# A fused linear attention, routed experts and a feed-forward layer: scatters moved behind GpSimd's mask in three rounds, one sum of logits moved behind the queries

## What is computed

```
state = alpha[t] * state + k[t] (outer) v[t];   y[t] = q[t] @ state      # attention, per head
logits = normalised(x) @ normalised(emb).T / tau;   e = argmax(logits)
x = gate_weight * (relu(x @ w1[e]) @ w2[e])                              # one expert per token
h = x @ w_in;   out = where(h > 0, h, exp(min(h, 0)) - 1) @ w_out
```

## Time and profile before

| quantity | value |
|---|---|
| median of 3 runs | 894.9 us |
| the profiled execution: its time, and its span | 891.97 us, 890.3 us |
| PE busy | 867.2 us, 97% of the span |
| DVE, ACT, POOL busy | 49%, 37%, 32% of the span |
| granted TensorE clock | 0.998 of full speed |
| attention | from the start to about 166 us |
| first two expert tiles | about 166 to 190 us |

### The profile page before, as it was taken

One profiled execution on the slowest core, in us unless ns is written; L12 is line 12 of the kernel. 1 busy time (PEld: TensorE's weight loads), 2 busy tenths in 40 slices (PEclk: granted clock), 3 DMA queues, 4 the chain that ended last, 5 costly groups with the idle time before them and its releaser, 6 DMA issues. The chain is left out here.

```text
span 890.3 us, 16092 instructions
## 1 busy us (share of the span) xinstructions
PE 867.2 (97%) x5725; PEld 774.7 (87%) x5725; DVE 433.6 (49%) x810; ACT 326.7 (37%) x698; POOL 284.2 (32%) x276
## 2 busy tenths in 40 slices
PE   8999999899999999999999999999999999999996
PEld 6888887689989998998988989899989999899985
DVE  7889898752232232232226445445445445445442
ACT  4576667732223222222222323233223323233322
POOL 3235655464755574285517102002002002002001
PEclk9999999999999999999999999999999999999999
DMA  9976774778778878757517002002002002000001
GB/s 151 164 145 127 175 155 104 271 237 283 232 245 274 297 206 270 244 153 212 161 54 234 16 1 72 0 1 72 1 1 72 1 1 72 1 0 31 7 1 36
DMA packets 140575, 106.35 MB, mean 119 GB/s; under 512 B 103338, under 2 KB 129058, under 8 KB 140498
## 3 DMA queue, kind: packets, MB, share of 16 engines
q0 software_dynamic: 24896, 62.95, 22.3%
q1 hardware_dynamic: 115602, 42.37, 21.3%
HBM read 87.94 MB, written 17.35 MB: 118 GB/s over the span
## 5 line engine op out<-in xcount | busy, mean ns | idle before, releaser
L1463 POOL DMA_INDIRECT out<-of,idi x24 | 26.8, 1115 | 364.0 <-ACT of L1569 300.8
L1276 PE MATMUL bank<-WX,hdTh 128*128 (+1 forms) x496 | 128.7, 340 | 0.5 <-PEq L448 0.5
L1505 PE MATMUL bank<-xT_h,wi_h 128*128 128x512 f32 x288 | 114.1, 396 | 0.0
L1505 PE MATMUL bank<-xT_l,wi_h 128*128 128x512 f32 x288 | 113.6, 395 | 0.0
L1505 PE MATMUL bank<-xT_h,wi_l 128*128 128x512 f32 x288 | 113.3, 393 | 0.0
L1575 ACT ACTIVATE ee<-bank 128x512 f32<-128x512 f32 x96 | 57.5, 599 | 146.7 <-PE bank L1505 144.6
L1597 DVE TENSOR_SCALAR em<-ee 128x512 f32<-128x512 f32 x96 | 44.2, 460 | 136.3 <-ACT ee L1575 134.8
L1260 PE MATMUL bank<-WX,xdTh 128*128 (+1 forms) x372 | 99.7, 403 | 3.6 <-ACT xdTh L1304 2.0
L1578 ACT ACTIVATE g_h<-gg 128x512 fp32r<-128x512 f32 x96 | 60.7, 632 | 114.9 <-DVE gg L1602 113.2
L1195 POOL TENSOR_TENSOR WX<-raw_w,WX 128x3072 fp32r<-128x3072 f32 x14 | 95.6, 6830 | 15.9 <-DMA WX<-moe_w 12.6
L1606 DVE TENSOR_TENSOR g_l<-gg,g_h 128x512 fp32r<-128x512 f32 x96 | 68.5, 713 | 60.3 <-ACT g_h L1578 59.4
(11 more groups left out here) (215 smaller groups left out, 1442.0 us busy)
## 6 DMA issues: line engine op xcount, KB each, us to landing
WX<-moe_w POOLq DMA_DIRECT2D x13, 1536.0 KB, 9.8
raw_w<-moe_w POOLq DMA_DIRECT2D x13, 1536.0 KB, 7.7
xd<-sorted_x SPq DMA_DIRECT2D x31, 193.0 KB, 5.3
sorted_y<-yd SPq DMA_DIRECT2D x31, 192.5 KB, 4.1
xg<-sorted_y SPq DMA_DIRECT2D x6, 770.0 KB, 4.6
nat_a<-alpha SPq DMA_DIRECT2D x32, 144.0 KB, 4.2
nat_k<-k SPq DMA_DIRECT2D x32, 144.0 KB, 3.5
nat_q<-q SPq DMA_DIRECT2D x32, 144.0 KB, 4.5
```

The costliest lines, as they stand in the source:

```text
L1276: last = pe.matmul(y_out(t)[:, 0:DM], hdT[a][:, k * P:(k + 1) * P], WX[:, bass.ds(off + (b * WE + KD * F + k * DM), DM)], start=(k == 0 an ...
L1505: last = pe.matmul(bank[4 + i % 2][:, :], a[:, k, w], b[:, k, :], start=(k == 0 and m == 0), stop=(k == KD - 1 and m == 2))
```

## The change

In rounds 8 and 12, three scatters stood between `Gm` and the mask `M1`. Now one stands there, and the other two behind `Zm`, which is behind `M1`. In round 14, two scatters stood ahead of `M1`; now one does, and five are behind `Gm` instead of four. In round 14 DVE adds the logits of pair 13 behind `Qh1` of pair 15 instead of between `Kh1` and the states. PE, ACT and SP keep their order.

```
             if n == PAIRS - 2:
-                out_ = [("M0", n)] + [(x, n + 1) for x in ("G", "Kh0", "Kh1")] + [("LA", n - 1)] + sums
-                out_ += [(x, n + 1) for x in ("R", "F", "Qh0", "Qh1")] + [("Y8", PARTIAL - 1)]
+                out_ = [("M0", n)] + [(x, n + 1) for x in ("G", "Kh0", "Kh1")] + sums
+                out_ += [(x, n + 1) for x in ("R", "F", "Qh0", "Qh1")] + [("LA", n - 1), ("Y8", PARTIAL - 1)]
...
                 elif b == PARTIAL - 1 and r == 2:
...
-                    out_[0:0] = [("SC", b * C + j) for j in range(2)]
-                    out_ += [("SC", b * C + j) for j in range(2, C)] + [(f"X{i}", b) for i in range(X_STEPS)]
+                    out_[0:0] = [("SC", b * C)]
+                    out_ += [("SC", b * C + j) for j in range(1, C)] + [(f"X{i}", b) for i in range(X_STEPS)]
...
                 elif b < PARTIAL - 1 and r == 4:
                     i = place_of(out_, "M1")
-                    out_[i:i] = [("SC", b * C + j) for j in range(HC, C)]
+                    out_[i:i] = [("SC", b * C + HC)]
+                    i = place_of(out_, "Zm") + 1
+                    out_[i:i] = [("SC", b * C + j) for j in range(HC + 1, C)]
```

## The result

The changed kernel takes 899.87 us (median of five runs, 898.46 to 900.37); the kernel before took 895.15 us beside it (five runs, 894.73 to 895.42). The ratio is 1.0046, with a 95% interval from 1.0036 to 1.0057. The prediction was 893.1 us, between 892.0 and 895.1, with a chance of 0.04 for slower. It was wrong in sign: the measured change is a loss of 4.7 us by the medians and of 4.1 by the ratio.

What follows compares the result with a forecast made beforehand. TensorE, busy 97% of the span, was taken as the bound, with gains only from its waits or later starts. Terms of 0.61, 0.53 and 0.67 us took the median from 894.9 to 893.1 us, range 892.0 to 895.1.

Steps and rivals of the forecast that it cites:

- I count the wait of round 14 and `LA` at nothing for the end: Round 14: removing PE's wait for the mask and moving the logits' sum were counted as no gain at the end.
- attention may end earlier without moving it: The expert phase hangs on batch 2's last scatter (160.16 us), so attention ending earlier does not shift it.
- Rounds 8 and 12 (-0.61, -0.53): From `KV` to the next `KT`, PE gets back its mask waits: 0.61 us in round 8, 0.53 in round 12.
- Round 14, mask and `LA`: Mask, held by `G`, ends at 153.54 instead of 154.55; `F` starts at 155.40 instead of 156.06.
- The last scatter of batch 2 (-0.67): Round 14: third scatter passes ahead of `F`, fourth is held, the last starts at 159.49, 0.67 us earlier.
- caught by `F`: Rival: `F` holds round 14's third scatter, the last starts 0.59 us later; 894.35 us, chance 0.26.
- that of the second scatter: Rival: states and `F` keep out round 14's second scatter, the last starts 1.85 us later; 895.6 us, chance 0.08.
- the wait of about 3 us that I took as room for the gain: ACT idles 3.06 us for a weight DMA ahead of `Wc`; 0.67 of it goes, so the shift has room.

Runs made afterwards that it cites:

- before again: The kernel before, unchanged, profiled a second time: 895.49 us (11 runs), ratio 1.0002, span 893.9.
- `LA` alone: Only the sum of the logits of pair 13 moved behind the queries, against the kernel before: 895.31 us (11 runs), ratio 0.9999.
- the run that was to part the two: The changed kernel with 24 more matmuls on TensorE between `KT0` and `A0` of pair 15: 898.6 us (7 runs), ratio 1.004.

## Why the prediction was wrong

**The step that failed.** "I count the wait of round 14 and `LA` at nothing for the end", together with "attention may end earlier without moving it". The prediction followed moved scatters only into GpSimd's queue, `Gm` and the token loads, and gave the hand-offs from TensorE to the other engines no cost. The runs show 3.89 us from `KT` of pair 15 to `A` instead of 1.39, and 3.59 us more from `A` to the first expert tile, and all of it with round 14's scatters.

**Rounds 8 and 12 (-0.61, -0.53).** The steps were right up to the mask: it starts inside `F`, is held (1.66 and 1.65 us; I expected about 1.9), and no `Yi1` waits. The size was mis-read from one execution. In the second profile of before, `KV` to `KT` takes 3.65 us in both rounds already (97.31 to 100.96, 137.22 to 140.87), with no wait for the mask: there is nothing to give back at that place. The time is lost earlier, at ACT's copy `C1`. Round 8 in the second profile of before, and in the changed kernel:

```profile
93.62 0.81 ACT L956 ACTIVATE asb<-bank 128x768 f32<-128x768 f32 x1 [2.07 <-PE bank L713]
```

```profile
92.85 0.81 ACT L958 ACTIVATE asb<-bank 128x768 f32<-128x768 f32 x1 [1.34 <-PE bank L658]
```

In the second profile of before, two scatters of round 8 run freely between `Gm` and `F` (91.50 and 92.79, `F` at 93.02), and `C1` starts 1.07 us behind the end of `A`. In the changed kernel one does, and it is 0.33. This is lateness again. It holds in both rounds of every profile: `C1` waits 2.04 to 2.15 us in the three with two free scatters there (before again, round 14's scatters alone, `LA` alone), and 1.05 to 1.61 in the ten in which the change leaves one. The first profile of before had one free scatter too, because `F` held the second (92.73, 2.20 us), and waited 1.33.

The change moves the two scatters to where ACT waits for the states. In the changed kernel `KV` to `KT` takes 5.11 us in round 8 (95.62 to 100.73) and 4.37 in round 12 (135.66 to 140.03), not 3.6: ACT's states start 1.57 and 0.80 us behind the end of `KV`, with the moved scatters running (95.87 and 97.18, 135.90 and 137.21), and `Ys` waits for them or for DVE. Round 11, where nothing was moved, takes 4.37 in the changed kernel and 4.21 in the second profile of before, against 3.60 in the earlier trace rows. In all, against that second profile, scan `G` of round 14 starts 0.84 us earlier in the changed kernel (153.72 against 154.56), where 1.14 was forecast.

**Round 14, mask and `LA`.** Right in size: the mask ends 0.67 us after `G` (154.44 + 1.69 against 155.46; predicted 0.66), and `F` starts 4.27 us behind `G` (153.72 to 157.99) instead of 4.93 in the second profile of before: 0.66 earlier, as predicted. Most of it comes from the mask: with the scatters of round 14 alone and `LA` still ahead of the states, it is 4.35 (154.55 to 158.90). What fell is that this counts for nothing at the end. I asked what `Yi1` and `F` gain, not what moving a scatter between the scans does to everybody else.

**The last scatter of batch 2 (-0.67).** Right in mechanism: the third scatter passes, 0.22 us ahead of `F` (157.77 and 157.99, predicted 0.23), the fourth is held (159.03 + 1.48 = 160.51, 0.76 us behind `F`'s end; predicted 0.77), and the last starts 8.37 us behind `G` instead of 9.02 (162.09; 163.58 in the second profile of before), 0.65 us earlier. So the rival "caught by `F`" did not happen, nor that of the second scatter, which took 0.99. With the 0.84 us of the rounds ahead the last scatter is 1.49 us earlier, and the token loads follow: 165.01 instead of 166.56, 1.55 us earlier where 1.81 was forecast. But "attention may end earlier without moving it" had an unspoken other half: attention may not end *later*. It did. `Wc` starts at 177.16 without any wait for the DMA; the wait of about 3 us that I took as room for the gain was consumed by attention.

**What made it slower** was none of the rivals. In the second profile of before, `F` held one scatter for its whole length:

```profile
159.60 2.41 POOL L1050 DMA_INDIRECT sorted_x<-xb,slot  x1 [0.30 <-issue]
```

So there one scatter (158.31) runs freely between the mask and `F`. In the changed kernel two do, because the third now starts just ahead of `F`, which is exactly what the term of -0.67 counted as its gain. PE's steps `Ys`, `Tq`, `KT` of round 14 are then seen late, while `F` is over. The loss by rows: from `KT` of pair 15 to `A` 3.89 us instead of 1.39, +2.50. From `A` to the first expert tile 14.08 instead of 10.49, +3.59; of this 2.5 us are `A` (2.93 against 1.61), `KV` (1.31 against 0.79) and `YN` (1.65 against 0.94) at the low clock. Less the 1.49 us by which `KT` came earlier (159.08 against 160.57), the first expert tile is 4.60 later. The span is 3.5 longer: PE's wait of 1.1 us for ACT in that tile, which the second profile of before has, is gone.

**What is shown and what isn't.** Shown: the loss is all in round 14's scatters (1.0042 alone, 0.9997 without them). With at most one scatter running freely between the mask and `F` the stall ahead of `A` doesn't arise (both profiles of before, the change without round 14, the scatters of rounds 8 and 12 alone, `LA` alone, the two variants that hold or delay the third, and the two that move all five away); with two it does (five kernels); and with the third held, the lateness follows the scatters to their new place (two kernels). TensorE's earlier arrival is not the cause: in all of these `KT` starts 1.08 to 1.14 us behind `F`, stall or not. By single runs: taking the weight load away doesn't remove the stall, and plain transfers of the same rows don't bring it. Only argued: how much of the loss would go if the clock stayed up, since the run that was to part the two missed. Open: why scatters that follow each other delay what others see of TensorE, and why the first profile of before was spared in rounds 7 and 11, with the same scatters at the same times (two free ones, 86.29 and 87.84, against 86.35 and 87.89). So the number of free scatters alone doesn't decide it everywhere. Whether TensorE's signal itself is late or its last writes are can't be told from rows that say "remote". Not tried: scatters further apart in rounds 7 to 12, where the lateness stands in before as well.

## What to carry to other kernels

An operation that is blocked may be doing the others a service: before filling the gap ahead of a long vector operation with one more indirect DMA, ask which cross-engine hand-offs of TensorE fall into that stretch, and whether they have the slack to come late (up to 2.7 us later here). Take a second profile of the kernel before when the first lies away from the median, 2.9 us here, which was more than the whole forecast gain; the steps that differ between the two are those on which no term should rest. And where a phase waits for data, its slack is also what the phase ahead may lose before it counts: write down both directions.

## What was not expected of the hardware

- Scatters that follow each other at 1.27 us (0.96 busy, 0.30 idle) go with hand-offs from TensorE to ScalarE and VectorE that come late: in the changed kernel waits of 2.62 us for `Qh0` and of 1.75 and 1.05 for `yT`, and 2.65 for the states with the third scatter held, all for steps that PE's rows show as done. Plain transfers of the same rows, at a DMA share of 0.96, didn't do so in one run.
- In all fourteen profiles a mask that starts inside a scan ends 0.65 to 0.68 us after it, and a scatter 0.76 to 0.78. The prediction put them at 0.66 and 0.77. The Trainium skill (SBUF — State Buffer, "Who interferes with whom") infers that writing descriptors is not hindered by a VectorE `tensor_tensor` with both inputs in SBUF. The prediction read this for scans too, and for a scan the measurement decides against that: the scatter of 159.60 took 2.41 us inside `F` in the second profile of before, and the next one, outside, 0.96.
- The same section says that of two operations that want the shared ports, the one that issues first blocks the other. For a mask and a scan the rows agree: behind a mask that started 0.16 us earlier the scan was stretched to 2.32 us. For a scatter they agree only by half: the third scatter, 0.22 us ahead of `F`, was not held (0.96), but `F` behind it was not either (1.76 us).
- 3.19 us without work on TensorE were followed by a granted clock of 0.66, 0.50 and 0.82 in the next stretches of 5 us. With 2.27 us of idle time it was 0.83 over 10 us.
